# Every other tile of the last block: last Newton step on GpSimd, its quotient fed unsplit to float32 products

## What is computed

```python
x = causal_conv(x, softmax(weight))        # 7 taps for each channel
h = x @ w_in;  x = (h * clip(h + 3, 0, 6) / 6) @ w_out          # layer 1, 192 -> 2048 -> 192
h = x @ w_in2
P = a0 + a1*h + a2*h*h + a3*h*h*h
Q = 1 + |b0|*|h| + |b1|*h*h
y = (P / (Q + 1e-6)) @ w_out2                                   # layer 2, 192 -> 2048 -> 192
```

## Time and profile before

| | us |
|---|---|
| median of 3 runs | 1205.32 (1204.94 to 1205.32) |
| the profiled execution, its own time | 1205.52 |
| its span in the trace | 1203.7 |
| granted TensorE clock, mean | 0.999 |

### The profile page before, as it was taken

The page is one execution under the profiler, slowest core; times in us unless marked ns, Lnnn a source line. Parts: engine busy times, 40 slices in busy tenths (PEclk is TensorE's granted clock), DMA queues, the critical chain, the costliest instruction groups (busy, mean ns, idle before and its releaser), DMA issues.

```text
span 1203.7 us, 18353 instructions
## 1 busy us (share of the span) xinstructions
PE 1181.9 (98%) x5154; PEld 966.3 (80%) x5154; DVE 1162.2 (97%) x1782; ACT 1171.1 (97%) x2238; POOL 1078.9 (90%) x834
## 2 busy tenths in 40 slices
PE   8999999999999999999999999999999999999987
PEld 6778888888888888888888888888888888888764
DVE  7899999999999999999999999999999999999898
ACT  8899999999999999999999999999999999999998
POOL 6889989999999999999898998999989999998876
PEclk9999999999999999999999999999999999999999
DMA  4400000000001000010000000000000000000000
GB/s 149 150 1 10 7 16 1 23 10 23 1 1 32 1 23 1 1 32 1 23 1 23 10 1 23 1 24 10 1 23 1 23 1 14 1 1 14 1 14 13
DMA packets 10021, 21.17 MB, mean 18 GB/s; under 512 B 1600, under 2 KB 1856, under 8 KB 9920
## 3 DMA queue, kind: packets, MB, share of 16 engines
q1 hardware_dynamic: 9632, 20.00, 5.6%
q10 hardware_dynamic: 288, 0.01, 0.0%
HBM read 13.72 MB, written 6.29 MB: 17 GB/s over the span
## 4 chain that ended last, share of the span: by engine, by line
PE 85%; ACT 5%; DVE 5%; issue 3%; POOL 0%; DMA 0%; ACTq 0%; DVEq 0%; POOLq 0%
PE h L326 43%; PE y0b_acc L343 4%; PE y0a_acc L338 4%; PE y0b_acc L344 4%; PE y0a_acc L340 4%; PE y0a_acc L339 4%; PE y1a_acc L338 4%; PE y1b_acc L344 4%; PE y1b_acc L343 4%; PE y1a_acc L339 4%; PE y1a_acc L340 4%; ACT g_hi L542 1%; DVE g L513 1%; DVE num L468 1%; ACT num L450 1%
## 5 line engine op out<-in xcount | busy, mean ns | idle before, releaser
L479 POOL TENSOR_TENSOR den<-den,sqr 128x512 f32<-128x512 f32 x246 | 359.0, 1459 | 91.3 <-ACT den L456 87.0
L536 POOL TENSOR_TENSOR g_lo<-g,g_hi 128x512 fp32r<-128x512 f32 x255 | 333.6, 1308 | 2.8 <-ACT g_hi L542 2.8
L443 POOL TENSOR_TENSOR g_lo<-r,g_hi 128x512 fp32r<-128x512 f32 x235 | 307.0, 1306 | 5.5 <-ACT g_hi L542 3.6
L473 DVE SCALAR_TENSOR_TENSOR num<-num,coef,h 128x512 f32<-128x512 f32 x246 | 183.9, 748 | 8.2
L506 DVE SCALAR_TENSOR_TENSOR h<-num,coef,h 128x512 f32<-128x512 f32 x238 | 178.6, 750 | 0.2
L468 DVE TENSOR_TENSOR num<-num,h 128x512 f32<-128x512 f32 x246 | 168.3, 684 | 10.3 <-ACT num L450 4.1
L450 ACT ACTIVATE num<-h,coef 128x512 f32<-128x512 f32 x246 | 176.3, 717 | 0.2
L542 ACT ACTIVATE g_hi<-g 128x512 fp32r<-128x512 f32 x255 | 167.9, 658 | 1.9 <-DVE g L513 0.4
L483 ACT ACTIVATE rsq<-den 128x512 f32<-128x512 f32 x246 | 158.7, 645 | 10.7 <-POOL den L479 7.7
L429 DVE SCALAR_TENSOR_TENSOR r<-r,h 128x512 f32<-128x512 f32 x235 | 160.9, 685 | 4.8 <-ACT r L422 3.6
L499 DVE SCALAR_TENSOR_TENSOR den<-den,h 128x512 f32<-128x512 f32 x238 | 162.1, 681 | 0.6 <-ACT h L495 0.3
(11 more groups left out here) (153 smaller groups left out, 2994.1 us busy)
## 6 DMA issues: line engine op xcount, KB each, us to landing
stage_w<-w_pack SPq DMA_DIRECT2D x16, 448.0 KB, 3.4
raw_a<-x_a SPq DMA_DIRECT2D x16, 259.0 KB, 3.2
out<-y_a SPq DMA_DIRECT2D x16, 256.0 KB, 2.0
out<-y_b SPq DMA_DIRECT2D x16, 128.0 KB, 2.3
raw_b<-x_b SPq DMA_DIRECT2D x14, 129.5 KB, 2.7
raw_b<-x_b SPq DMA_DIRECT2D x4, 65.5 KB, 4.5
tap_ab<-taps ACTq DMA_DIRECT2D x1, 7.0 KB, 3.1
coef<-coefs ACTq DMA_DIRECT2D x1, 3.0 KB, 2.9
```

Of the source, the lines that this page charges most:

```text
L443: eng.tensor_tensor(g1_lo[t % 2][:, :], gated(t)[:, :], f32(g1_hi[t % 2][:, :]), ALU.subtract).then_inc(S["g1lo"], 1)
L473: eng.scalar_tensor_tensor(out=n, in0=n, scalar=a1, in1=h2_of(t), op0=ALU.add, op1=ALU.mult).then_inc(S["num1"], 1)
L479: eng.tensor_tensor(den_of(t), den_of(t), sqr_of(t), ALU.add).then_inc(S["den_sum"], 1)
L536: eng.tensor_tensor(g2_lo[t % 2][:, :], g2[t % 2][:, :], f32(g2_hi[t % 2][:, :]), ALU.subtract).then_inc(S["g2lo"], 1)
```

## The change

Seven tiles of the last block, t = 241, 243, ..., 253, are "full" (`FULL` counts them back from the last). For a full tile:

- `g_first` writes its result over the numerator in SBUF instead of over the reciprocal in PSUM, as only the last tile did before.
- `g_neg` is issued by POOL instead of DVE, as two instructions: den - 2, then (after a wait on the first one's semaphore) times the quotient, into `g`.
- `g2hi` (ACT) and `g2lo` (POOL) are left out.
- The out-product is two matmuls of float32 operands: the raw weights `w_full` times `g`, 128 columns of weights for the first output channels, 64 for the others.
- The raw weights of the seven tiles come by seven DMAs of 128x192 float32 (`load_w_full`), issued on SP ahead of the store of block 14, into five buffers that are no longer in use.

What waited for `g_neg` of a tile waits for `g_full` or `g_done` according to the tile (`wait_g`). The counts of `g_done`, `g2hi`, `g2lo` skip the full tiles (`splits`).

Beside this, the extra layer-2 step moves from p = 233 to p = 251, and the tables TURN and END have new orders and lags (in END, `sq2` is issued a step ahead, the out-product a tile earlier than before, the in-product three tiles further ahead; on POOL the order is `g2lo`, `den_sum`, `g_neg`).

```diff
-EXTRA = (233,)
+EXTRA = (251,)
 END = {
-    "tensor": [("in2", 1), ("out2", 5)],
-    "scalar": [("rsq2", 1), ("x2b_hi", SUM1, 1), ("abs2", 0), ("sq2", 0), ("y1a_out", SUM1, -2), ("rec2", 1),
-             ("y2a_out", SUM2, -1), ("g2hi", 2), ("lin2", 0), ("y2b_move", SUM2, -2), ("x2a_hi", SUM1, -2)],
-    "vector": [("num2", 1), ("g2lo", 3), ("x2b_res", SUM1, 3), ("x2b_lo", SUM1, 5), ("y2b_sum", SUM2, -1),
-             ("g_neg", 2), ("num1", 1), ("newton", 1), ("g_first", 1)],
-    "gpsimd": [("g2lo", 3), ("den_sum", 0), ("x2a_lo", SUM1, 1)],
+    "tensor": [("out2", 4), ("in2", -2)],
+    "scalar": [("abs2", 0), ("x2b_hi", SUM1, -1), ("x2a_hi", SUM1, -1), ("y2a_out", SUM2, -1), ("rsq2", 1),
+             ("sq2", -1), ("y1a_out", SUM1, -1), ("rec2", 1), ("g2hi", 2), ("lin2", 0), ("y2b_move", SUM2, -2)],
+    "vector": [("y2b_sum", SUM2, -1), ("x2b_lo", SUM1, 4), ("x2b_res", SUM1, 2), ("num2", 1), ("g_neg", 2),
+             ("g2lo", 3), ("num1", 1), ("newton", 1), ("g_first", 1)],
+    "gpsimd": [("g2lo", 3), ("den_sum", 0), ("x2a_lo", SUM1, 2), ("g_neg", 2)],
 }
 TURN = {
-    "tensor": [("out2", 4), ("in2", -2)],
+    "tensor": [("out2", 4), ("in2", -1)],
...
+FULL = (2, 4, 6, 8, 10, 12, 14)
...
+        full = sorted(NT - 1 - i for i in FULL)
+        spent = [r1[0], r1[1], y_a[0], raw_a[1], x2b_rest]
+        w_full = {t: spent[i // 2][:, i % 2 * (DA + DB):(i % 2 + 1) * (DA + DB)] for i, t in enumerate(full)}
...
         def raw_quotient(t):
-            return quotient(t) if t < NT - 1 else num_of(t)
+            return num_of(t) if t in full or t == NT - 1 else quotient(t)
...
+            if t in full:
+                eng.wait_ge(d_w_full, 16 * len(full))
+                wait_g(eng, t)
+                w, g = w_full[t], g2[t % 2][:, :]
+                eng.matmul(ya_acc[1][:, :], w[:, 0:DA], g, start=False, stop=False)
+                eng.matmul(yb_acc[1][0:DB, :], w[:, DA:DA + DB], g, start=False, stop=False) \
+                    .then_inc(S["n2_done"], 1)
+                spare_products(eng, t)
+                return
...
         def rec2(eng, t):
...
-                eng.wait_ge(S["g_done"], t - 1)
+                wait_g(eng, t - 2)
...
         def g_neg(eng, t):
+            if (t in full) != (eng is nc.gpsimd):
+                return
             eng.wait_ge(S["newton"], t + 1)
             eng.wait_ge(S["g_first"], t + 1)
-            after(eng, S["g2lo"], t - 1)
...
+            if t - 2 in full:
+                eng.wait_ge(S["n2_done"], t - 1)
+            else:
+                after(eng, S["g2lo"], splits(t - 2))
+            if eng is nc.gpsimd:
+                eng.tensor_scalar(den_of(t), den_of(t), 2.0, None, ALU.subtract).then_inc(S["less_two"], 1)
+                eng.wait_ge(S["less_two"], fulls(t))
+                eng.tensor_tensor(g2[t % 2][:, :], den_of(t), raw_quotient(t), ALU.mult) \
+                    .then_inc(S["g_full"], 1)
...
         def g2hi(eng, t):
+            if t in full:
+                return
             after(eng, S["n2_done"], t - 1)
...
+        def load_w_full(eng):
+            for name, count in (("g1lo", NT), ("x2a_lo", NB), ("conv_a_tap", K * NB), ("x2b_lo", NB)):
+                eng.wait_ge(S[name], count)
+            for t in full:
+                f = t % NF
+                at = in_cols + f % WCHUNK * (DA + DB)
+                eng.dma_start(w_full[t], w_pack[1, f // WCHUNK, :, at:at + DA + DB]).then_inc(d_w_full, 16)
+
         def store_y(eng, k):
+            if k == NB - 2:
+                load_w_full(eng)
```

More of the change, by code:

```diff
@@ L97 @@
     "sync": [("store_y", SUM2, 1)],
-    "tensor": [("out2", 4), ("in2", -2)],
[L99 to L103, removed]
+    "tensor": [("out2", 4), ("in2", -1)],
+    "scalar": [("y1a_out", SUM1, 0), ("rsq2", 1), ("x2a_hi", SUM1, 0), ("y2a_out", SUM2, 0), ("abs2", 0),
+             ("sq2", 0), ("rec2", 1), ("x2b_hi", SUM1, -3), ("lin2", 0), ("g2hi", 2), ("y2b_move", SUM2, 0)],
+    "vector": [("g2lo", 6), ("num2", 1), ("num1", 1), ("y2b_sum", SUM2, -2), ("x2b_res", SUM1, 0),
+             ("x2b_lo", SUM1, -1), ("g_neg", 2), ("newton", 1), ("g_first", 1)],
+    "gpsimd": [("x2a_lo", SUM1, -5), ("g_neg", 2), ("den_sum", 0), ("g2lo", 2)],
 }
@@ L253, in quotient, with fulls, splits, wait_g @@
             return ([ya_acc[0], yb_acc[0]][t % 2] if t >= SPARE else h_banks[bank2[t]])[:, :]
+        full = sorted(NT - 1 - i for i in FULL)
+        spent = [r1[0], r1[1], y_a[0], raw_a[1], x2b_rest]
+        w_full = {t: spent[i // 2][:, i % 2 * (DA + DB):(i % 2 + 1) * (DA + DB)] for i, t in enumerate(full)}
+        def fulls(t):
+            return sum(u <= t for u in full)
+        def splits(t):
+            return t + 1 - fulls(t)
+        def wait_g(eng, t):
+            if t in full:
+                eng.wait_ge(S["g_full"], fulls(t))
+            elif t >= 0:
+                eng.wait_ge(S["g_done"], splits(t))
         def raw_quotient(t):
-            return quotient(t) if t < NT - 1 else num_of(t)
+            return num_of(t) if t in full or t == NT - 1 else quotient(t)
         def den_of(t):
@@ L274, in wait_buffer @@
                     eng.wait_ge(S[name], count)
+            elif used == "g_done":
+                wait_g(eng, t - 4)
             else:
                 eng.wait_ge(S[used], t - 3)
+                if used == "g_first" and t - 4 in full:
+                    wait_g(eng, t - 4)
         d_raw = [sem(f"d_raw{i}") for i in range(2)]
@@ L281, in build_program @@
         d_w = [sem(f"d_w{i}") for i in range(W_STAGES)]
+        d_w_full = sem("d_w_full")
         d_const, d_tap, d_out_a, d_out_b = (sem(n) for n in ("d_const", "d_tap", "d_out_a", "d_out_b"))
         names = """h1_done relu1 gate1 g1hi g1lo n1_done
-                   h2_done lin2 abs2 sq2 num2 num1 den_sum rsq_done rec newton g_first g_done
+                   h2_done lin2 abs2 sq2 num2 num1 den_sum rsq_done rec newton g_first g_done less_two g_full
                    g2hi g2lo n2_done n2a_done
@@ L388, in pe_out2 @@
                 eng.wait_ge(S["g1lo"], EARLY)
+            if t in full:
[7 more added lines that the diff above has]
+                return
             if t < NT - 2:
-                eng.wait_ge(S["g2lo"], t + 1)
+                eng.wait_ge(S["g2lo"], splits(t))
                 out_product(eng, 1, t, g2_hi[t % 2], g2_lo[t % 2], ("y2a_out", "y2b_sum")) \
@@ L402, in pe_out2 @@
             yb = yb_last if last else yb_acc[1][:, :]
-            eng.wait_ge(S["g2hi"], t + 1)
+            eng.wait_ge(S["g2hi"], splits(t))
             eng.matmul(ya_acc[1][:, :], a_hi, g_hi[:, :], start=False, stop=False)
@@ L509, in g_neg @@
         def g_neg(eng, t):
+            if (t in full) != (eng is nc.gpsimd):
+                return
             eng.wait_ge(S["newton"], t + 1)
             eng.wait_ge(S["g_first"], t + 1)
-            after(eng, S["g2lo"], t - 1)
-            eng.scalar_tensor_tensor(out=g2[t % 2][:, :], in0=den_of(t), scalar=2.0,
-                                     in1=raw_quotient(t), op0=ALU.subtract, op1=ALU.mult) \
-               .then_inc(S["g_done"], 1)
+            if t - 2 in full:
[7 more added lines that the diff above has]
+                    .then_inc(S["g_full"], 1)
+            else:
+                eng.scalar_tensor_tensor(out=g2[t % 2][:, :], in0=den_of(t), scalar=2.0,
+                                         in1=raw_quotient(t), op0=ALU.subtract, op1=ALU.mult) \
+                   .then_inc(S["g_done"], 1)
         def g2hi(eng, t):
+            if t in full:
+                return
             after(eng, S["n2_done"], t - 1)
             if t < NT - 1:
-                eng.wait_ge(S["g_done"], t + 1)
+                wait_g(eng, t)
                 ins = round_hi(eng, g2_hi[t % 2][:, :], g2[t % 2][:, :])
@@ L529, in g2lo @@
         def g2lo(eng, t):
-            if (t == NT - 1) != (eng is nc.vector):
+            if t in full or (t == NT - 1) != (eng is nc.vector):
                 return
-            eng.wait_ge(S["g2hi"], t + 1)
+            eng.wait_ge(S["g2hi"], splits(t))
             if t == NT - 1:
-                eng.wait_ge(S["g_done"], NT)
-                eng.wait_ge(S["g2lo"], t)
+                wait_g(eng, t)
+                eng.wait_ge(S["g2lo"], splits(t - 1))
             eng.tensor_tensor(g2_lo[t % 2][:, :], g2[t % 2][:, :],
```

## The result

| | before | after |
|---|---|---|
| median of 9 runs each, one chip, us | 1205.32 (1204.94 to 1205.43) | 1208.6 (1208.47 to 1208.92) |
| ratio, 95% interval | | 1.0028 (1.0018 to 1.0038) |
| the profiled execution | 1205.52 | 1208.92 |
| its span | 1203.7 | 1207.1 |
| granted TensorE clock, mean | 0.999 | 0.999 |

A forecast was written before the change was run, and what follows sets the result against it. The prediction held ACT and DVE, both full in the last block at 6.23 us a pair, to be the bound. POOL pacing at 5.89, the extra step's 0.3 and 0.65 given back in the tail made 1.8 gained: 1203.5, range 1201.8 to 1206.3.

The forecast's parts named there:

- the price of the subtraction on POOL: Last block, each full tile: one-input subtraction between 0.52 and 1.29 us, taken as 0.75, plus 0.1 for the product's wait.
- The wait: Last block: `rec2` waits for the full tile two before; the loop closes at POOL's 5.89 us a pair, no wait added.
- G: End of a full tile's product on POOL; `rec2` two tiles later starts 0.05 after; for tile 253 forecast 1193.1.
- POOL as the fullest engine: Last block: POOL needs 5.89 us a pair of tiles and paces, ahead of ACT's 5.70.
- The first full tile: Start of the sequence: POOL, walked from tile 241 on, ends the product of tile 243 at 1163.95.
- The extra step and the turn: Extra step from p = 233 to 251: 0.3 us gained, bounds 0 and 0.6; new orders and seven loads cost nothing.
- The float32 product: Out-product on PE: four passes with hidden weight loads, 0.91 us each; PE at 5.2 us a pair stays below ACT.
- The end: After tile 253's product PE works without a gap for 5.35 us, last matmul at 1198.45; tail gives back 0.65.
- C: Rival: subtraction costs 1.29 like an addition, POOL needs 6.43 a pair, 1.5 us slower, 1206.8; chance 0.15.
- D: Rival: PE becomes the bound, float32 products at 1.68 make pairs of 6.77, 4.4 us slower, 1209.7; chance 0.08.
- A: Main case: POOL paces the last block with a subtraction of 0.65 to 0.95, 1203.0 to 1204.8 us; chance 0.50.
- B: Rival: subtraction costs only 0.52 to 0.6, ACT paces with 5.70 a pair, 1201.7 to 1202.4 us; chance 0.20.

The follow-up runs named there:

- e6: Changed kernel with the subtraction of 2 issued by DVE after `g_first`, POOL only multiplying: 1204.72 against 1204.91 for the kernel before, ratio 0.9998.
- e7: Changed kernel with `rec2` waiting on `newton` and `g_first` of a full tile instead of its last step: 1207.46 against 1204.94 for the kernel before.
- e8: Changed kernel with only four full tiles, 243, 246, 249 and 252: 1206.72 against 1204.91 for the kernel before, ratio 1.0017.
- e1: Changed kernel without POOL's subtraction of 2 (full tiles wrong in value): 1202.63 against 1204.94 for the kernel before, ratio 0.9981.
- e5: Changed kernel with the subtraction as a two-input tensor_tensor against a buffer of twos: 1206.89 against 1204.94 for the kernel before, ratio 1.0016.
- e4: Kernel before with only the extra layer-2 step moved from p = 233 to 251: 1204.49 against 1204.91, ratio 0.9996.
- e3: Changed kernel with no full tile, only the new orders and the moved extra step: 1204.83 against 1204.94 for the kernel before, ratio 1.0000.
- e10: Changed kernel with full tiles 243, 246, 249, 252 only and `rec2` waiting on `newton` and `g_first`: 1206.56 against 1205.24 for the kernel before.
- e12: Changed kernel without each full tile's second float32 product (64 weight columns; output incomplete): 1207.84 against 1205.24 for the kernel before, ratio 1.0022.
- e13: Changed kernel, subtraction on DVE (241, 245, 249, 253) or ACT (243, 247, 251), `rec2` waiting on `newton` and `g_first`: 1204.75 against 1204.92 for the kernel before.
- e11: Changed kernel with tile 253 split again, six full tiles instead of seven: 1207.64 against 1205.24 for the kernel before, ratio 1.0023.

## Why the prediction was wrong

**The step that failed is the price of the subtraction on POOL.** "So one input lies between 0.52 and 1.29 ... I take 0.75." The rows gave two kinds of instruction, a write without input and an addition of two tensors, and I put a third kind between them by its number of inputs. It took 1.49, above the upper bound. Start to start it is 1.57 where 0.85 (0.75 and the wait of 0.1) had been reckoned. With 5 pairs from tile 243 to 253 that is 5 x 0.72 = 3.6 us of the 4.85 by which the product of tile 253 ended late (1197.95 for 1193.1). The Trainium skill, GPSIMD Engine Reference, "Engine selection", calls one-input elementwise work there "roughly line-rate"; the trace disagrees for this form, 1.49 us on POOL against 0.56 on DVE (e6).

**The wait.** "So the loop closes at POOL's own 5.89 and no wait is added on top" was walked with a margin of 0.06 us between `g2hi` and POOL's need of it. It came 0.14 late in each pair: `rec2` began at G + 0.10 and not 0.05, while POOL, which starts an instruction some 0.05 before the recorded end of the one before, was ready for `g2lo` at G + 1.19. e7 puts it at 0.15 a pair, 0.7 us by pair 253 and 0.8 in the time. In e8, where POOL has slack, the same wait paces outright. So the statement that it adds nothing was the second thing wrong, a smaller one in the change as it is. A margin of 0.06 in a walk of ten steps, each known to some hundredths, was no ground to write zero.

**POOL as the fullest engine** was right, and so were its signs: POOL busy 19.48 of 20 us, ACT idle before every second `rec2` with POOL's product as the releaser, PE with time to spare. That was partly luck: by the forecast's own numbers POOL led ACT by only 0.19, and it leads clearly because the price is twice what I took. At the measured price the same sum gives 5.04 + 1.57 = 6.61 a pair, and with the wait's 0.14 it is 6.75 (6.68 measured, since the additions and the product are 1.23 to 1.27 from start to start, 4.97 together). e1 and e5 bear out the rest of the sum: from e5 (+1.95, with 1.37 from start to start) down to the 0.85 that I had reckoned is 7 x 0.52 = 3.6 us, an estimate of some 1.7 below before; forecast was 1.8.

**The first full tile.** Its product ended at 1164.27, forecast 1163.95 less the 0.3 of the extra step: 0.62 late, for which the 0.72 of its own subtraction is enough.

**The extra step and the turn.** `rec2`(243) came 0.51 earlier and e4 shows 0.4 for the step alone; forecast 0.3, bounds 0 and 0.6. No gap stands after p = 233 nor after p = 251. The orders cost nothing, as said (e3), and the seven loads, issued from 1140.8 to 1144.0, land in 2.1 us each, well before the first product that needs them.

**The float32 product** was taken at 0.91 by four passes; it is 1.02, some 4.5 times the 0.227 of an fp32r product (nine of them take 2.04 from 1161.03 on). That is 0.1 each and 0.2 of the tail (product of 253 to last matmul 5.65 us, forecast 5.35).

**The end was missed.** The last pair took 6.94, not 6.68. PE stood idle for 2.08 us before the out-product of tile 251, and ran it slowly (PE, POOL and the stretch of the changed kernel):

```profile
1191.14 1.85 PE L419 MATMUL y1a_acc<-g,y_a 128*128 128x512 f32 x2 [2.08 <-POOL g L556]
1192.92 1.97 PE L420 MATMUL y1b_acc<-g,y_a 128*64 128x512 f32 x2
```

```profile
1195.08 1.49 POOL L554 TENSOR_SCALAR den<-den 128x512 f32<-128x512 f32 x1 [0.25 <-PE y1b_acc L420]
```

```profile
1186.00:1200.00 14.00, 11.49 (x31) 4.87 (x29) 12.17 (x19) 9.83 (x19) 12.17 (x10) 0.88 0.00 1
```

The granted clock is 0.88 over these 14 us, against 1.00 in the same stretch of the kernel before, and 0.50 from 1192 to 1194. The lower of its two levels, 1.2 GHz, would double 1.02 to 2.04, and the rows show 1.85 and 1.97. POOL's subtraction of tile 253 waited 0.25 for the second of them. In the change most of the slow products hides behind POOL, which is later still; in e10 it does not.

So the 4.85 by which the product of tile 253 was late are 3.6 for the price, 0.7 for the wait, 0.62 for the first full tile and 0.25 for the end, less some 0.35 for POOL's other work (4.97 a pair for 5.04).

**The rivals.** C named the right mechanism (POOL dearer than an addition's worth makes the pair longer) and stopped at 1.29: 1.5 above before. e5, whose instruction is just that, came to 1.95 above. D, PE as the bound, would have given 4.4 above before, near the measured 3.3 for the wrong reason; e12 rules it out. A and B fall with the price. The chance of C was too low for a form of instruction of which no row existed, and its end should have lain open above the two-input price.

## What to carry to other kernels

Where a change moves work to a third engine because two are full, its gain hangs on the price of the moved instruction in exactly its form: an instruction that isn't in the trace has no upper bound in a neighbour with more inputs, and measuring that one form (tensor_scalar on POOL, 1.49 us) would have decided this case before anything else. Sum the receiving engine's period first with the dearest plausible price; here 5.04 us of other work left it 1.2 us until it became slower than the pair of 6.23. And 7.0 us of visible waiting of ACT for POOL was worth 0.8 us when taken away (e7), while the instruction that filled POOL was worth 5.6 (e1): look first for what keeps the releaser busy. Where the releaser has idle time of its own, as in e8, the wait itself can be what paces.

## What the runs showed of the hardware

- POOL, 128x512 float32 in SBUF: tensor_scalar in place 1.48 to 1.50 us, tensor_tensor 1.27 to 1.30, both in the same stretch. The same tensor_scalar on DVE: 0.56, or 0.48 from start to start. ACT's copy with a bias: 0.64.
- While DVE's tensor_scalar runs, POOL's addition beside it takes 1.49 instead of 1.30 (e6), and in e13, where it begins 0.57 before the addition instead of 0.23, DVE's instruction takes 0.89 instead of 0.56 as well (the addition 1.47). The Trainium skill, GPSIMD Engine Reference, "Specifications", lists GpSimd's SBUF interfaces as shared with VectorE, with contention for some kinds of VectorE instructions. Which kind this one is, the rows don't tell; what the two cost each other is from these rows.
- A float32 matmul of 128x512 is recorded as two, costs 1.02 to 1.03 us from start to start with 128 columns of weights against 0.23 in fp32r, and hardly less, 1.00, with 64.
- The granted clock fell to its lower level around out-products that PE had waited for 1.85 (e5), 1.95 (e7), 2.04 (e10) and 2.08 us (the change), and did not in the profiles of e8 and e11 after 2.04 and 2.06 us, nor in e12 after 2.72 and 2.04 us. So the idle time alone doesn't tell; what does was not found. The two groups of runs of e8, e10 and e11 go with the mean clock on record, and their medians lie 1.2 to 1.3 us apart. In the change, whose runs lie within 0.45 us of each other, the clock on record (0.998 to 1.000) does not go with the time.
